# A recurrence, two expert layers and one core: the layout of its chunks in SBUF, its running products and its warming products

## The chip, the cores and the metric

The kernel runs on one core of a Trainium2 chip. The metric is the device time of one execution in microseconds. Three executions of the kernel before gave 916.23, 917.78 and 918.56 us, so the median is 917.78 us.

## The reference

For 4 batches of 8 heads a state of 48 by 48 is carried over 768 time steps with a complex gate for each row, and read by q:

```
mag = sqrt(a_re^2 + a_im^2);  scale = min(mag, 0.999) / (mag + 1e-6)
a_re, a_im = a_re * scale, a_im * scale                # B,H,S,D = 4,8,768,48
for t in range(S):
    S_re, S_im = ar*S_re - ai*S_im + k[t] v[t]^T, ar*S_im + ai*S_re
    y[t] = q[t] @ S_re
x = y as 3072 rows of 384
e = argmax(x @ w_gate + modality_bias[modality_id])     # one of 8 experts
x = gate_w * (relu(x @ w1[e]) @ w2[e])                  # 384 -> 1024 -> 384
out = (((x @ mid_w1) * (x @ mid_w2)) @ w3) @ w_out
```

## The kernel before, in words

**Stages.** First the gates are scaled. Then the recurrence is turned into products of matrices over chunks of CH = 128 time steps, 24 chunks of tokens with all their heads: the running product p(t) of the gates within a chunk is formed, q is multiplied by p(t) and k by 1/p(t). After that, for each chunk, TensorE forms scores (k times q, L1347), VectorE masks them with a causal triangle (L1253), and TensorE adds scores times v (L1397) and the state that came into the chunk (L1401). The rows then go through the gate and, sorted by expert, through the expert layers and the second layer, which is TensorE work from about 388 us to the end.

**The running products.** The gates of all batches lie in `gates[P, 2, NG, ROW]`: 128 partitions, real and imaginary plane, NG = 12 groups, and in a row 6 chunks of PITCH = 130 words. A chunk is worked on as two halves of SUB = 64 steps at once, so that a loop of 63 steps does for all (`for u in range(SUB - 1)`, L1052). In step u VectorE multiplies the gate of step u + 1, both planes, by the running product of step u: L1056 by its real and L1057 by its imaginary part, 288 elements each into `prods`, and L1059 and L1060 combine the products into the new real and imaginary part, 144 elements each (12 groups, 6 chunks, 2 halves). L1059 and L1060 wait for the products, the next step for L1060. All stands on VectorE, one instruction behind the other.

**The layout before.** The host interleaves the halves (`by_step`): word 2j + h of a chunk is step j of half h, so that the two words that a step touches in a chunk are neighbours. Two pad words end a chunk. Row p of a tile of tokens is therefore token `(p % 2) * 64 + p // 2` of its chunk (`when`), for the mask, for v, for the modality ids and for the token numbers that go with the sorted rows.

**The joins.** Two stages per batch (`stages`, 12 and 6 of its 18 chunk rows) finish a chunk: `join` (L1070 on) multiplies the second half by the last product of the first. Its steps 0 and 1 issue two instructions each at L1080 (real plane, imaginary plane), step 2 combines (L1084, L1085) and copies the last word to the pads (L1089 for the first stage, L1091 for the others). `norm` and `finish` then form 1/p from |p|^2, with Square, Ln and Exp on ScalarE (L878, L883, L888), and multiply in k (L1119, L1122, L1124) and q (L1136, L1127, L1129).

**What sets the order.** Everything is written out by hand. VectorE does the joins and finishes of the first two stages before the chunk loop, and the later ones between the chunks (`prepare(b, slot)`). SyncE's queue copies the finished planes into `ks` and `qs` (`stack_k`, `stack_q`, L753 and L724), which the scores read. TensorE, before the loop, forms w3 times w_out (L1326, L1331), then waits for the first half of k (`k_half_ready`, given by L1122) and runs 8 products of constants (`keep_busy`, L1318) until `ks` and `qs` are there.

Of the kernel before, what the change touches and what calls it, by code (L numbers as in the profile page):

```python
# [37 lines left out]
def constants(n_experts, n_tiles, n_steps, D, n_in, n_hidden):  # L38
# [10 lines left out]
    when = (row % 2) * SUB + row // 2  # L49
    put("causal", (when[:, None] <= when[None, :]) * 1.0)  # L50
# [14 lines left out]
    put("token", when[:, None] + CH * np.arange(n_tiles)[None, :])  # L65
# [535 lines left out]
def attention(nc, sem, io, shapes, L, R, W):  # L601
# [24 lines left out]
    with ExitStack() as room:  # L626
# [7 lines left out]
        def cst(name, rows=P):  # L634
# [4 lines left out]
            "p (w c n h) -> p w c n h", w=2, c=2, h=2)  # L639
# [68 lines left out]
        def plane(x, b):  # L708
            return gates[:, x, b * GB:(b + 1) * GB].rearrange("p g (c t) -> p (g c) t", t=PITCH)[:, :, 0:CH]
# [115 lines left out]
        def scalar(act):  # L825
            act.wait_ge(filled, 1)

            def re_square(b):
                act.wait_ge(gates_in[b][RE], landed(b))
                nc.scalar.activation(mags[b][:, :, :], plane(RE, b), ACT.Square).then_inc(re_squared, 1)  # L830

            def im_square(b):
                act.wait_ge(gates_in[b][IM], landed(b))
                nc.scalar.activation(squares[b], plane(IM, b), ACT.Square).then_inc(im_squared, 1)
# [39 lines left out]
            def square(k, x):  # L874
                b, part = stages[k]
                act.wait_ge(joined, k + 1)
                out = (norms[b], seeds[b])[x]
                nc.scalar.activation(out[:, part], plane(x, b)[:, part], ACT.Square).then_inc(p_squared, 1)  # L878
# [131 lines left out]
        def vector(dve):  # L1010
            def im_square(b):
                dve.wait_ge(gates_in[b][IM], landed(b))
                nc.vector.tensor_tensor(squares[b], plane(IM, b), plane(IM, b), ALU.mult).then_inc(im_squared, 1)
# [12 lines left out]
            def scale(b):  # L1026
# [4 lines left out]
                for x in (RE, IM):  # L1031
                    ins = nc.vector.scalar_tensor_tensor(out=plane(x, b), in0=mags[b][:, :, :], scalar=1.0, in1=plane(x, b),  # L1032
                                                         op0=ALU.subtract, op1=ALU.mult, reverse0=True)
# [30 lines left out]
            def join(k, step):  # L1064

                b, part = stages[k]
                half = gates[:, :, b * GB:(b + 1) * GB].rearrange("p x g (c j h) -> p x (g c) h j", j=SUB + 1, h=2)[:, :, part]
# [8 lines left out]
                if step < 2:  # L1076
                    last = half[:, step, :, 0, SUB - 1:SUB].broadcast_to([P, part.stop - part.start, SUB])
                    out = (by_re, by_im)[step]
                    for x in (RE, IM):
                        ins = nc.vector.tensor_tensor(out[:, x], half[:, x, :, 1, 0:SUB], last, ALU.mult)  # L1080
                    ins.then_inc(halves_done, 1)
                else:
# [4 lines left out]
                    if k == 0:  # L1087
                        pads = L.early_q[:, :, :, :].rearrange("p x g (c t) -> p x (g c) t", t=PITCH)[:, :, :, CH:PITCH]
# [15 lines left out]
            def finish(k, step):  # L1104
# [15 lines left out]
                elif step == 3:  # L1120
                    dve.wait_ge(kinv_ready, k + 1)
                    nc.vector.tensor_tensor(seed, inv, plane(RE, b)[:, part], ALU.mult).then_inc(k_half_ready, 1)  # L1122
                elif step == 4:
                    nc.vector.tensor_tensor(inv, inv, plane(IM, b)[:, part], ALU.mult).then_inc(kt_ready, 1)  # L1124
                elif step == 5:
                    dve.wait_ge(q_loaded, (b + 1) * DMA)
                    nc.vector.tensor_tensor(plane(RE, b)[:, part], plane(RE, b)[:, part], q_in[:, part], ALU.mult)  # L1127
                else:
                    nc.vector.tensor_tensor(plane(IM, b)[:, part], plane(IM, b)[:, part], q_in[:, part],  # L1129
                                            ALU.mult).then_inc(qt_ready, 1)  # L1130

            def early_q():
                dve.wait_ge(q_loaded, DMA)
                for x in (RE, IM):
                    out = L.early_q[:, x].rearrange("p g (c t) -> p (g c) t", t=PITCH)[:, :, 0:CH]
                    nc.vector.tensor_tensor(out, plane(x, 0)[:, parts[0]], q_in[:, parts[0]], ALU.mult).then_inc(q_early_ready, 1)  # L1136
# [164 lines left out]
        def tensor(pe):  # L1301
# [4 lines left out]

            def turn_y(g):
# [28 lines left out]
            keep_busy(8, bank_scores[0])  # L1336

            for g in range(CHUNKS + 1):
# [3 lines left out]
                if g < CHUNKS:  # L1342
# [45 lines left out]
                if g:  # L1388
# [3 lines left out]
                    for pair in range(HU // 2):  # L1392
# [6 lines left out]
                        if last:  # L1399
                            for i, out, wide in zip(heads, outs, (HALF, D)):  # L1400
                                mm = nc.tensor.matmul(out, state[:, i * D:i * D + wide],  # L1401
                                                      qs[before % NU][:, i, last * PITCH:last * PITCH + CH], start=False, stop=True)
# [21 lines left out]
def recurrence(nc, sem, io, shapes, L, R, W):  # L1424
# [10 lines left out]
    with ExitStack() as room:  # L1435
# [36 lines left out]
        def sync(sp):  # L1472
            with sp.If(general(sp)):
# [29 lines left out]
                for b in range(B):  # L1503
                    for h in range(2):
                        sp.dma_start(L.rows(b)[h:P:2, :, 0:DM], io["x_rows"][b * S:(b + 1) * S, :].rearrange(
# [632 lines left out]
```

## Time and profile before

| | |
|---|---|
| median of 3 runs | 917.78 us |
| the profiled execution | 917.5 us, span 915.7 us |
| TensorE matmuls, busy | 768.6 us (84%) |
| VectorE, busy | 496.7 us (54%), 963 instructions |
| ScalarE, busy | 331.2 us (36%) |
| granted TensorE clock, mean | 0.966 |

The span is the time from the first to the last recorded instruction. Busy shares are means over stages in which different engines set the pace. A line such as L1056 is a line of the kernel before; "rows" and "gates" in the names of the profile are the buffers `rows0` (where `prods` lies) and `gates`, "mags" holds `norms` and `seeds`, "spare" k and q as loaded. TensorE's passes of fp32 products are recorded one by one, so that 8 products show as 16 rows.

### The profile page before, as it was taken

To read this page: it belongs to the slowest core of one execution; us is meant where nothing else is said; L and a number is where in the kernel's file an instruction comes from. 1 tells how busy PE (TensorE), PEld (TensorE's weight loads), DVE (VectorE), ACT (ScalarE), POOL (GpSimd) and SP (SyncE) were. 2 spreads that over 40 slices of the span, in tenths; PEclk is the share of its full clock that TensorE was granted. 3 is DMA by queue.
4 is the path that set the end of the run, shared out by engine and by line. 5 is a ranking of instruction groups with operands and counts; after the bars stand their busy time and mean duration, and the time that the engine had idled before them with its cause. 6 is when DMAs were issued, how large, how long until landed. Compare 5 with 4: busy or idle time off the path is not lost.

```text
span 915.7 us, 11775 instructions
## 1 busy us (share of the span) xinstructions
PE 768.6 (84%) x4541; PEld 641.9 (70%) x4541; DVE 496.7 (54%) x963; ACT 331.2 (36%) x657; POOL 128.7 (14%) x127
## 2 busy tenths in 40 slices
PE   0029910399999999899999999999999999999995
PEld 0015500188888888787888888888989898988885
DVE  4999999999899975866453454341111111212010
ACT  6932100354545434534453452333122222223120
POOL 0201100000000032410000000013232222323231
PEclk9999965599999999999999999999999999999998
DMA  9982120456666656427423430160000000000000
GB/s 380 373 270 83 69 87 0 122 147 172 185 180 165 188 161 206 141 81 238 147 96 104 128 106 9 73 207 1 35 0 35 1 26 9 18 18 9 26 1 35
DMA packets 46756, 99.19 MB, mean 108 GB/s; under 512 B 11616, under 2 KB 29920, under 8 KB 44384
## 3 DMA queue, kind: packets, MB, share of 16 engines
q1 hardware_dynamic: 41056, 79.37, 28.3%
q0 software_dynamic: 5632, 18.94, 5.9%
q8 instruction: 40, 0.66, 0.3%
q14 instruction: 28, 0.23, 0.1%
HBM read 60.32 MB, written 18.94 MB: 87 GB/s over the span
## 4 chain that ended last, share of the span: by engine, by line
PE 69%; DVE 19%; DMA 3%; ACT 3%; issue 2%; SPq 2%; POOL 1%; DVEq 0%
PE moe_bank L557 17%; PE moe_bank L558 17%; PE moe_bank L559 17%; PE bank L1347 4%; DVE rows L1056 3%; DVE rows L1057 3%; PE bank L1381 3%; DVE gates L1059 2%; PE bank L1397 2%; PE bank L1313 2%; DVE gates L1032 2%; DVE gates L1060 2%; DMA gates<-a_im 1%; PE bank L1401 1%; PE bank L1353 1%
## 5 line engine op out<-in xcount | busy, mean ns | idle before, releaser
L1934 DVE TENSOR_TENSOR u_sb<-x_in,moe_bank 128x512 f32<-128x512 f32 x48 | 33.0, 688 | 229.1 <-PE moe_bank L559 229.1
L1772 POOL TENSOR_TENSOR hid_lo<-u_sb,hid_hi 128x512 fp32r<-128x512 f32 x48 | 62.4, 1299 | 357.9 <-ACT hid_hi L1829 357.9
L557 PE MATMUL moe_bank<-xT_hi,w_hi 128*128 128x512 f32 x264 | 104.8, 397 | 0.0
L558 PE MATMUL moe_bank<-xT_lo,w_hi 128*128 128x512 f32 x264 | 104.8, 397 | 0.0
L559 PE MATMUL moe_bank<-xT_hi,w_lo 128*128 128x512 f32 x264 | 104.0, 394 | 0.0
L1326 PE MATMUL bank<-early_w_out,early_w3T 128*128 128x384 f32 x128 | 45.4, 512 | 66.3 <-DMA early_w_out<-w_out 62.9
L1326 PEld LDWEIGHTS bank<-early_w_out,early_w3T 128*128 128x128 f32 x128 | 24.9, 199 | 86.3 <-issue 65.0
L1848 ACT COPY x_in<-moe_bank 128x512 f32<-128x512 f32 x48 | 28.1, 586 | 143.7 <-PE moe_bank L559 143.7
L559 PE MATMUL moe_bank<-w_hi,hid_lo 128*128 128x384 f32 x192 | 64.5, 336 | 0.0
L557 PE MATMUL moe_bank<-w_hi,hid_hi 128*128 128x384 f32 x192 | 64.4, 335 | 0.0
L558 PE MATMUL moe_bank<-w_lo,hid_hi 128*128 128x384 f32 x192 | 64.4, 335 | 0.0
L559 PEld LDWEIGHTS moe_bank<-xT_hi,w_lo 128*128 128x128 f32 x264 | 49.9, 189 | 11.8
L557 PEld LDWEIGHTS moe_bank<-xT_hi,w_hi 128*128 128x128 f32 x264 | 49.5, 187 | 12.1 <-DVE hid_lo L552 0.4
L558 PEld LDWEIGHTS moe_bank<-xT_lo,w_hi 128*128 128x128 f32 x264 | 49.7, 188 | 11.5
L1318 PE MATMUL bank<-consts 128*128 128x512 f32 x16 | 9.7, 772 | 56.3 <-DVE mags L1122 56.3
L559 PE MATMUL moe_bank<-xT_hi,m_lo 128*128 128x512 f32 x144 | 56.8, 394 | 0.0
L557 PE MATMUL moe_bank<-xT_hi,m_hi 128*128 128x512 f32 x144 | 56.7, 393 | 0.0
L558 PE MATMUL moe_bank<-xT_lo,m_hi 128*128 128x512 f32 x144 | 56.6, 393 | 0.0
L1347 PE MATMUL bank<-qs,ks 96*128 96x128 f32 x384 | 55.4, 287 | 1.3 <-DMA qs<-gates 1.3
L1347 PEld LDWEIGHTS bank<-qs,ks 96*128 96x128 f32 x384 | 46.6, 191 | 9.2 <-issue 7.7
L557 PE MATMUL moe_bank<-hid_hi,w_hi 128*128 128x512 f32 x128 | 51.0, 398 | 0.0
L558 PE MATMUL moe_bank<-hid_lo,w_hi 128*128 128x512 f32 x128 | 50.2, 393 | 0.0
(219 smaller groups left out, 1641.1 us busy)
## 6 DMA issues: line engine op xcount, KB each, us to landing
stage<-w SPq DMA_DIRECT2D x10, 1536.0 KB, 8.3
ks<-mags SPq DMA_DIRECT2D x48, 144.0 KB, 2.8
x_sorted<-early_zero POOLq DMA_DIRECT2D x8, 772.0 KB, 21.9
qs<-gates SPq DMA_DIRECT2D x40, 146.2 KB, 2.7
gates<-a_re SPq DMA_DIRECT2D x4, 1170.0 KB, 12.3
gates<-a_im SPq DMA_DIRECT2D x4, 1170.0 KB, 14.7
x_in<-x_sorted SPq DMA_DIRECT2D x24, 193.0 KB, 3.0
spare<-k SPq DMA_DIRECT2D x4, 1152.0 KB, 5.4
```

Of the source, the lines that this page charges most:

```text
L557: nc.tensor.matmul(out, l_hi, r_hi, start=first, stop=False)
L558: nc.tensor.matmul(out, l_hi, r_lo, start=False, stop=False)
L559: return nc.tensor.matmul(out, l_lo, r_hi, start=False, stop=last)
L1032: ins = nc.vector.scalar_tensor_tensor(out=plane(x, b), in0=mags[b][:, :, :], scalar=1.0, in1=plane(x, b), op0=ALU.subtract, op1=ALU.mult, ...
L1056: nc.vector.tensor_tensor(prods[:, 0], at[:, :, :, u + 1], re, ALU.mult)
L1057: nc.vector.tensor_tensor(prods[:, 1], at[:, :, :, u + 1], im, ALU.mult).then_inc(products, 1)
L1326: mm = nc.tensor.matmul(psum[f % 2][:, 0:DM], L.w3T[:, k, f * P:(f + 1) * P], L.w_out[:, k], start=(k == 0), stop=True, skip_group_check=True)
L1347: mm = nc.tensor.matmul(bank_scores[g % 2][:, i * CH:(i + 1) * CH], ks[m][:, i, c * CH:(c + 1) * CH], qs[m][:, i, c * PITCH:c * PITCH + CH ...
L1381: mm = nc.tensor.matmul(bank_s[0:SD, i * WIDE:(i + 1) * WIDE], krs[last % 2][:, i], v_flat[:, at:at + WIDE], start=(last == 0 and i == 0), ...
L1772: nc.gpsimd.tensor_tensor(hid_lo[:, f], u_sb[:, f % 2], hid_hi[:, f].bitcast(F32), ALU.subtract).then_inc(u_lo_ready, 1)
L1848: nc.scalar.copy(a_sb[:, f % 2], bank_a[f % 2][:, :]).then_inc(a_ready, 1)
L1934: nc.vector.tensor_tensor(u_sb[:, f % 2], a_sb[:, f % 2], bank_b[f % 2][:, :], ALU.mult).then_inc(u_ready, 1)
```

## The change

**Layout.** The host no longer interleaves. A chunk is its two halves in the order of time, each followed by one pad word (64 + 1 + 64 + 1 words, 130 as before), so row p of a tile is token p of its chunk. `plane` gives runs of 64 words where it gave runs of 128, and `halved` and `of_halves` bring the other operands into the same shape. The word that step u touches is now alone: 144 words per plane, 65 words (260 bytes) apart. The scores and the state products read `qs` as two runs of 64 (`chunk_of_q`).

**One instruction for the products.** The products by the real and by the imaginary part become one instruction of 576 elements with both operands broadcast. In a join the two planes of step 0 become one instruction, and so do those of step 1.

**Six warming products** in place of eight.

```
-    when = (row % 2) * SUB + row // 2
-    put("causal", (when[:, None] <= when[None, :]) * 1.0)
+    put("causal", (row[:, None] <= row[None, :]) * 1.0)
...
         def plane(x, b):
-            return gates[:, x, b * GB:(b + 1) * GB].rearrange("p g (c t) -> p (g c) t", t=PITCH)[:, :, 0:CH]
+            return gates[:, x, b * GB:(b + 1) * GB].rearrange("p g (r t) -> p (g r) t", t=SUB + 1)[:, :, 0:SUB]
+
+        def halved(a):
+            return a.rearrange("p c (h t) -> p (c h) t", h=2)
+
+        def of_halves(part):
+            return slice(2 * part.start, 2 * part.stop)
...
-            at = gates[:, :, :, :].rearrange("p x g (c j h) -> p x (g c) j h", j=SUB + 1, h=2)
+            at = gates[:, :, :, :].rearrange("p x g (r j) -> p x (g r) j", j=SUB + 1)
+            both = [P, 2, 2, NG * BLK]
             for u in range(SUB - 1):
-                re, im = (at[:, x:x + 1, :, u].broadcast_to([P, 2, NG * NCH, 2]) for x in (RE, IM))
                 if u:
                     dve.wait_ge(prefix_step, u)
-                nc.vector.tensor_tensor(prods[:, 0], at[:, :, :, u + 1], re, ALU.mult)
-                nc.vector.tensor_tensor(prods[:, 1], at[:, :, :, u + 1], im, ALU.mult).then_inc(products, 1)
+                nc.vector.tensor_tensor(prods, at[:, :, :, u + 1].unsqueeze(1).broadcast_to(both),
+                                        at[:, :, :, u].unsqueeze(2).broadcast_to(both), ALU.mult).then_inc(products, 1)
                 dve.wait_ge(products, u + 1)
                 nc.vector.tensor_tensor(at[:, RE, :, u + 1], prods[:, 0, 0], prods[:, 1, 1], ALU.subtract)
                 nc.vector.tensor_tensor(at[:, IM, :, u + 1], prods[:, 0, 1], prods[:, 1, 0],
                                         ALU.add).then_inc(prefix_step, 1)
...
-                half = gates[:, :, b * GB:(b + 1) * GB].rearrange("p x g (c j h) -> p x (g c) h j", j=SUB + 1, h=2)[:, :, part]
+                half = gates[:, :, b * GB:(b + 1) * GB].rearrange("p x g (c h j) -> p x (g c) h j", j=SUB + 1, h=2)[:, :, part]
...
-                    last = half[:, step, :, 0, SUB - 1:SUB].broadcast_to([P, part.stop - part.start, SUB])
+                    last = half[:, step:step + 1, :, 0, SUB - 1:SUB].broadcast_to([P, 2, part.stop - part.start, SUB])
                     out = (by_re, by_im)[step]
-                    for x in (RE, IM):
-                        ins = nc.vector.tensor_tensor(out[:, x], half[:, x, :, 1, 0:SUB], last, ALU.mult)
-                    ins.then_inc(halves_done, 1)
+                    nc.vector.tensor_tensor(out, half[:, :, :, 1, 0:SUB], last, ALU.mult).then_inc(halves_done, 1)
...
-                        pads = L.early_q[:, :, :, :].rearrange("p x g (c t) -> p x (g c) t", t=PITCH)[:, :, :, CH:PITCH]
+                        pads = L.early_q[:, :, :, :].rearrange("p x g (c h j) -> p x (g c) h j", j=SUB + 1, h=2)[:, :, :, :, SUB]
...
+            def chunk_of_q(m, i, c):
+                return qs[m][:, i, c * PITCH:(c + 1) * PITCH].rearrange("p (h t) -> p h t", h=2)[:, :, 0:SUB]
...
-            keep_busy(8, bank_scores[0])
+            keep_busy(6, bank_scores[0])
...
-                        mm = nc.tensor.matmul(bank_scores[g % 2][:, i * CH:(i + 1) * CH], ks[m][:, i, c * CH:(c + 1) * CH],
-                                              qs[m][:, i, c * PITCH:c * PITCH + CH], start=True, stop=True)
+                        mm = nc.tensor.matmul(bank_scores[g % 2][:, i * CH:(i + 1) * CH].rearrange("p (h t) -> p h t", h=2), ks[m][:, i, c * CH:(c + 1) * CH],
+                                              chunk_of_q(m, i, c), start=True, stop=True)
...
-        chunks = np.pad(by_step(a).reshape(P, -1, S // CH, CH), ((0, 0), (0, 0), (0, 0), (0, 2)))
-        return np.ascontiguousarray(chunks).reshape(P, -1, S // CH * (CH + 2))
+        halves = np.pad(packed(a).reshape(P, -1, S // SUB, SUB), ((0, 0), (0, 0), (0, 0), (0, 1)))
+        return np.ascontiguousarray(halves).reshape(P, -1, S // SUB * (SUB + 1))
```

On VectorE, the last step of the running products, the first two stages' joins and what stands between them, in the kernel before ("rows" is `prods`; the numbers are partitions and free sizes of what is written):

```order
L1056 TENSOR_TENSOR rows<-gates 128x288
L1057 TENSOR_TENSOR rows<-gates 128x288
L1059 TENSOR_TENSOR gates<-rows 128x72x2
L1060 TENSOR_TENSOR gates<-rows 128x72x2
L1080 TENSOR_TENSOR mags<-gates 128x12x64 x4
L1084 TENSOR_TENSOR gates<-mags 128x12x64
L1085 TENSOR_TENSOR gates<-mags 128x12x64
L1089 COPY early_q<-gates 128x24x2
L1136 TENSOR_TENSOR early_q<-gates,spare 128x12x128 x2
L1098 SCALAR_TENSOR_TENSOR mags<-mags 128x1536
L1102 TENSOR_REDUCE guard<-mags 128x1
L1080 TENSOR_TENSOR mags<-gates 128x6x64 x4
```

And the same piece after the change (its lines have moved: L1061 is the products, L1064 and L1065 combine them, L1084 is the join):

```order
L1061 TENSOR_TENSOR rows<-gates 128x576
L1064 TENSOR_TENSOR gates<-rows 128x144
L1065 TENSOR_TENSOR gates<-rows 128x144
L1084 TENSOR_TENSOR mags<-gates 128x2x12x64 x2
L1087 TENSOR_TENSOR gates<-mags 128x12x64
L1088 TENSOR_TENSOR gates<-mags 128x12x64
L1092 COPY early_q<-gates 128x48
L1140 TENSOR_TENSOR early_q<-gates,spare 128x24x64 x2
L1101 SCALAR_TENSOR_TENSOR mags<-mags 128x1536
L1105 TENSOR_REDUCE guard<-mags 128x1
L1084 TENSOR_TENSOR mags<-gates 128x2x6x64 x2
```

Nothing has changed its place; a step has three instructions where it had four, a join four where it had six, and the combining ones write 144 single words where they wrote 72 pairs.

On TensorE, the end of the work before the chunk loop and its first rows, before the change (L1318 is the warming product, L1347 the scores):

```order
L1331 MATMUL bank<-early_minus,consts 128x384 x2
L1318 MATMUL bank<-consts 128x512 x8
L1347 MATMUL bank<-qs,ks 128x128 x4
L1361 MATMUL bank<-qs,consts 96x24 x2
L1372 MATMUL bank<-consts,ks 128x96 x4
```

And after it (L1326 is the warming product, L1355 the scores):

```order
L1339 MATMUL bank<-early_minus,consts 128x384 x2
L1326 MATMUL bank<-consts 128x512 x6
L1355 MATMUL bank<-qs,ks 128x128 x4
L1369 MATMUL bank<-qs,consts 96x24 x2
L1380 MATMUL bank<-consts,ks 128x96 x4
```

Two warming products are gone; the rest stands as it was.

## Rows read from the trace of the kernel before

**Rows 1.** The page's part 4, shares of the chain by engine:
```profile
PE 69%; DVE 19%; DMA 3%; ACT 3%; issue 2%; SPq 2%; POOL 1%; DVEq 0%
```
**Rows 2.** Stretches: length; busy PE, PEld, DVE, ACT, POOL; clock, DMA share, GB/s:
```profile
64.08:153.84 89.76, 49.71 (x143) 27.01 (x141) 85.42 (x252) 11.17 (x24) 8.59 (x16) 0.82 0.21 75
153.84:184.54 30.70, 9.51 (x16) 4.10 (x17) 30.28 (x33) 9.09 (x8) 0.00 (x0) 0.57 0.41 100
184.54:352.87 168.33, 159.91 (x1630) 142.17 (x1628) 148.21 (x282) 83.15 (x223) 9.04 (x7) 1.00 0.62 169
```
**Rows 3.** VectorE in order of time, the first step; start us, duration us:
```profile
64.08 0.46 DVE L1056 TENSOR_TENSOR rows<-gates 128x288 f32<-128x288 f32 x1
64.45 0.45 DVE L1057 TENSOR_TENSOR rows<-gates 128x288 f32<-128x288 f32 x1
64.94 0.31 DVE L1059 TENSOR_TENSOR gates<-rows 128x144 f32<-128x144 f32 x1
65.17 0.30 DVE L1060 TENSOR_TENSOR gates<-rows 128x144 f32<-128x144 f32 x1
65.50 0.46 DVE L1056 TENSOR_TENSOR rows<-gates 128x288 f32<-128x288 f32 x1
```
**Rows 4.** VectorE by shape; busy us, mean ns of one, idle before:
```profile
L1056 DVE TENSOR_TENSOR rows<-gates 128x288 f32<-128x288 f32 x63 | 28.9, 458 | 2.2
L1059 DVE TENSOR_TENSOR gates<-rows 128x144 f32<-128x144 f32 x63 | 19.5, 309 | 2.2
L1080 DVE TENSOR_TENSOR mags<-gates 128x768 f32<-128x768 f32 x16 | 14.5, 948 | 0.0
```
**Rows 5.** VectorE by shape, reduces and one-source instructions, dense and strided:
```profile
L1022 DVE TENSOR_SCALAR mags<-mags 128x2304 f32<-128x2304 f32 x3 | 4.1, 1355 | 0.1
...
L254 DVE TENSOR_REDUCE route_c<-route_work 128x6 f32<-128x48 f32 x12 | 2.4, 200 | 0.3
...
L254 DVE TENSOR_REDUCE route_work<-part 128x48 f32<-128x192 f32 x3 | 1.4, 480 | 0.0
...
L1102 DVE TENSOR_REDUCE guard<-mags 128x1 f32<-128x12 f32 x4 | 0.7, 174 | 0.1
...
L254 DVE TENSOR_REDUCE route_c<-route_work 128x2 f32<-128x16 f32 x4 | 0.7, 167 | 0.1
L1102 DVE TENSOR_REDUCE guard<-mags 128x1 f32<-128x6 f32 x4 | 0.7, 163 | 0.1
...
L1091 DVE COPY gates<-gates 128x24 f32<-128x24 f32 x3 | 0.6, 191 | 0.1
...
L251 DVE TENSOR_SCALAR mod_f<-mod_f 128x24 f32<-128x24 f32 x2 | 0.4, 178 | 0.1
...
L254 DVE TENSOR_REDUCE route_work<-part 128x16 f32<-128x64 f32 x1 | 0.3, 267 | 0.0
...
L1089 DVE COPY early_q<-gates 128x48 f32<-128x48 f32 x1 | 0.2, 191 | 0.0
```
**Rows 6.** The chain in order of time, from 153 us: start us, us, what:
```profile
153.84 3.58 DVE mags L1080 x4
...
182.22 1.75 DVE mags L1080 x2
...
185.95 0.68 DVE scores L1253
```
**Rows 7.** TensorE's weight loads in order of time, in brackets the idle time before:
```profile
179.43 0.34 PEld L1318 LDWEIGHTS bank<-consts 128*128 128x128 f32 x1 [0.52 <-issue]
...
180.68 0.19 PEld L1318 LDWEIGHTS bank<-consts 128*128 128x128 f32 x1 [0.24 <-issue]
...
184.12 0.19 PEld L1347 LDWEIGHTS bank<-qs,ks 96*128 96x128 f32 x1 [0.24 <-issue]
```
**Rows 8.** SyncE's queue in order of time, the first planes of k:
```profile
174.91 6.23 SPq L753 DMA_DIRECT2D ks<-mags  x10
```
**Rows 9.** The transfers that write or read `ks`, 170 to 190 us:
```profile
DMA to landing us min/median/max: 2.2/2.8/3.2
```

More of the change, by code:

```diff
@@ L64, in constants @@
     put("region", one * (n_tiles * CH * np.arange(n_experts)))
-    put("token", when[:, None] + CH * np.arange(n_tiles)[None, :])
+    put("token", row[:, None] + CH * np.arange(n_tiles)[None, :])
     put("step", one * np.arange(n_steps))
@@ L829, in re_square @@
                 act.wait_ge(gates_in[b][RE], landed(b))
[L830 removed]
+                nc.scalar.activation(halved(mags[b][:, :, :]), plane(RE, b), ACT.Square).then_inc(re_squared, 1)
             def im_square(b):
                 act.wait_ge(gates_in[b][IM], landed(b))
[L834 removed]
+                nc.scalar.activation(halved(squares[b]), plane(IM, b), ACT.Square).then_inc(im_squared, 1)
             def root(b):
@@ L877, in square @@
                 out = (norms[b], seeds[b])[x]
-                nc.scalar.activation(out[:, part], plane(x, b)[:, part], ACT.Square).then_inc(p_squared, 1)
+                nc.scalar.activation(halved(out[:, part]), plane(x, b)[:, of_halves(part)], ACT.Square).then_inc(p_squared, 1)
             def log(k):
@@ L1012, in im_square @@
                 dve.wait_ge(gates_in[b][IM], landed(b))
-                nc.vector.tensor_tensor(squares[b], plane(IM, b), plane(IM, b), ALU.mult).then_inc(im_squared, 1)
+                nc.vector.tensor_tensor(halved(squares[b]), plane(IM, b), plane(IM, b), ALU.mult).then_inc(im_squared, 1)
             def add(b):
@@ L1031, in scale @@
                 for x in (RE, IM):
-                    ins = nc.vector.scalar_tensor_tensor(out=plane(x, b), in0=mags[b][:, :, :], scalar=1.0, in1=plane(x, b),
+                    ins = nc.vector.scalar_tensor_tensor(out=plane(x, b), in0=halved(mags[b][:, :, :]), scalar=1.0, in1=plane(x, b),
                                                          op0=ALU.subtract, op1=ALU.mult, reverse0=True)
@@ L1134, in early_q @@
                 for x in (RE, IM):
-                    out = L.early_q[:, x].rearrange("p g (c t) -> p (g c) t", t=PITCH)[:, :, 0:CH]
-                    nc.vector.tensor_tensor(out, plane(x, 0)[:, parts[0]], q_in[:, parts[0]], ALU.mult).then_inc(q_early_ready, 1)
+                    out = L.early_q[:, x].rearrange("p g (r t) -> p (g r) t", t=SUB + 1)[:, :, 0:SUB]
+                    nc.vector.tensor_tensor(out, plane(x, 0)[:, of_halves(parts[0])], halved(q_in[:, parts[0]]),
+                                            ALU.mult).then_inc(q_early_ready, 1)
             for step in range(3):
@@ L1400, in tensor @@
                             for i, out, wide in zip(heads, outs, (HALF, D)):
-                                mm = nc.tensor.matmul(out, state[:, i * D:i * D + wide],
-                                                      qs[before % NU][:, i, last * PITCH:last * PITCH + CH], start=False, stop=True)
+                                mm = nc.tensor.matmul(out.rearrange("p (h t) -> p h t", h=2), state[:, i * D:i * D + wide],
+                                                      chunk_of_q(before % NU, i, last), start=False, stop=True)
                     mm.then_inc(yT_psum, 1)
@@ L1504, in sync @@
                     for h in range(2):
-                        sp.dma_start(L.rows(b)[h:P:2, :, 0:DM], io["x_rows"][b * S:(b + 1) * S, :].rearrange(
+                        sp.dma_start(L.rows(b)[h * SUB:(h + 1) * SUB, :, 0:DM], io["x_rows"][b * S:(b + 1) * S, :].rearrange(
                             "(c h j) v -> h j c v", h=2, j=SUB)[h]).then_inc(rows_back, DMA)
@@ L2113 @@
     arrays = {
-        "a_re": spaced(a_re), "a_im": spaced(a_im), "k": by_step(k), "q_packed": by_step(q), "q": by_dim(q),
-        "v": np.ascontiguousarray(v.transpose(0, 2, 1, 3).reshape(NT, 2, SUB, H * D).transpose(2, 1, 0, 3)
-                                  ).reshape(CH, NT, H * D),
+        "a_re": spaced(a_re), "a_im": spaced(a_im), "k": packed(k), "q_packed": packed(q), "q": by_dim(q),
+        "v": np.ascontiguousarray(v.transpose(0, 2, 1, 3).reshape(NT, CH, H * D).transpose(1, 0, 2)),
         "a_re_d": by_dim(a_re), "a_im_d": by_dim(a_im), "k_d": by_dim(k),
```

17 lines of the change are left out of this document (8 added, 9 removed).

## The prediction

> **What bounds the kernel now.** I read the chain of waits first, since the change touches many lines and only those on the chain can move the end. TensorE holds 69% of it and VectorE 19% [rows 1]. The second view is the table of stretches: from 64.08 to 153.84 us VectorE is busy for 85.42 of 89.76 us, while TensorE does 49.71 us of other work that ends inside the stretch; ScalarE does 11.17 us and the DMA share is 0.21. After 184.54 TensorE is the full engine, 159.91 of 168.33 us [rows 2]. So the program has a VectorE part up to about 190 us and a TensorE part behind it, and every microsecond added to the VectorE part before the first scores moves everything behind it: the chunk loop cannot start without k and q, and nothing in it waits for anything else that is that early.
>
> The third view is the order of time on VectorE. In the running products the four instructions of one step start at 64.08, 64.45, 64.94 and 65.17, and the next step starts at 65.50 [rows 3]. The 63 steps end when the first join starts at 153.84 [rows 6]: (153.84 - 64.08) / 63 = 1.425 us per step. Nothing but VectorE itself stands between them.
>
> From these starts I take the cost of an instruction apart. 288 elements followed by an independent instruction take 0.37 to 0.38 us from start to start, 144 elements 0.23: about 1.04 ns an element and 0.075 us besides. Where the next instruction waits for the result, it is 0.49 for 288 and 0.33 for 144, so some 0.19 us besides. The means by shape agree: 458 ns for 288 elements and 309 for 144 give 1.035 ns an element, and a duration of 150 ns plus 1.04 ns an element gives 949 for 768, where 948 stands [rows 4].
>
> **The running products, if only the count of elements mattered.** Two instructions of 288 become one of 576 and the two of 144 stay. The new step is 576 x 1.04 + 190 = 0.789, then 0.225, then 0.335: 1.349 us, which is 0.076 less than 1.425, and 63 times that is -4.8 us. This is what the edit in the order of instructions is worth by itself.
>
> **The running products, with the new layout.** The other half of the edit is what the elements are. Before, the two halves of a chunk were interleaved, so each step read and wrote pairs of neighbouring words, one pair every 520 bytes. After, step u touches one word every 260 bytes. In these rows pairs pay nothing: 288 elements in pairs take 458 ns, where that formula gives 450 [rows 4]. Single words far apart are in the trace in three places [rows 5]:
> - The reduce of `part`, whose inner reads lie 32 bytes apart, takes 480 ns for 192 elements and 267 for 64: 1.66 ns an element. The reduces of the dense `route_work` take 200 ns for 48 and 167 for 16, 1.03 ns an element.
> - The reduce for `guard` reads one word every 512 bytes: 174 ns for 12 and 163 for 6, so 1.83 ns an element.
> - The one-source copy L1091 reads and writes one word every 520 bytes: 191 ns for 24 words, where a dense one-source instruction of 24 elements takes 178. Dense, such instructions run at (1355 - 178) / (2304 - 24) = 0.52 ns an element (L1022); the 13 ns more for 24 lone words add 0.54, so a lone word costs twice a dense one. At two elements side by side that is about 2.1 ns for each, which I round to 2.0. L1089 writes 48 words in pairs, each source word read twice, in 191 ns too: pairs pay nothing here either.
>
> So a lone word costs 1.66 to 2.0 ns where a dense one costs 1.04. What no row shows is a two-source instruction with both sources lone, nor a lone write with dense reads, which is what the two instructions that combine the products will do. I bound each:
> - The product instruction: 190 + 576 x 1.66, 1.83 or 2.0 = 1.146, 1.244 or 1.342 us from start to start, provided that the two source streams run beside each other as they do now. The lower bound is the 0.789 of the dense case; the upper one, if the two streams must take turns, is 190 + 576 x 3.66 = 2.298.
> - The two combining instructions: 0.56 us together if writes are free of it, 0.075 + 0.185 + 288 x r = 0.74, 0.79 or 0.84 if a lone write pays like a lone read. The copy L1091 has both kinds and cannot tell them apart.
>
> I take r = 1.83, since the reads of the `guard` reduce are the nearest in spacing and are read in the one-element-at-a-time form, and I take it for the writes too, because L1091, with lone reads and lone writes, pays the most of the three (2.0). The step is then 1.244 + 0.787 = 2.031 us, +0.606, and 63 steps are +38.2 us. Reads alone would be 1.244 + 0.56 = 1.804, +23.9 us.
>
> The Trainium skill speaks to this twice and the two passages pull apart. "Advanced Engine Details and Errata", section "SBUF Cachelines", says that SBUF works in lines of 16 bytes and that at least two hits on a line are needed to hide its latency; a pair is exactly two hits, a lone word one. The three places above agree with it. "VectorE: DVE Perf Modes", section "Mode 1× (REGULAR) — the baseline", says of the plain mode of two-source fp32 instructions that odd strides simply work in it, because nothing is packed; read as a promise of speed, it gives the -4.8 us of the dense case. The `guard` and `part` reduces read slower with stride here, so I give it little weight.
>
> **The joins.** Four instructions per join become two, each twice as long, so per join two gaps of 0.075 us go. Their halves are now dense runs of 64 where they were every second word; the row of every second word already runs at the dense price, 948 ns for 768 [rows 4], so the layout brings nothing there. On the chain before 190 us lie the four of the first join, the four of the second and two pairs of the third; the first four and the last pair stand in [rows 6]. That is six gaps, -0.45 us. The later joins lie beside TensorE's work; nothing.
>
> **The other layout edits.** Scaling and squares now work on 36 runs of 64 for 18 runs of 128, the matmuls that read `qs` on two runs of 64: the same elements, dense, 0. The pad copy of 48 words becomes lone writes, at most 48 x 0.5 = 24 ns, nothing. The constants, v and the modality ids are rearranged on the host at equal size.
>
> **Six warming products for eight.** Each has two passes, so sixteen in all. A weight load and the idle time before it make 0.34 + 0.52 = 0.86 us a pass at 179.43, and 0.19 + 0.24 = 0.43 at 180.68; the load for the first scores starts at 184.12 [rows 7]. In the stretch from 153.84 to 184.54 the mean granted clock is 0.57, and 1.00 after it [rows 2]: the passes run at 1.2 GHz first, and at 2.4 from somewhere between these two rows on. Six products are twelve passes, so four fast ones, 4 x 0.43 = 1.7 us, go: TensorE would be free at 184.5 - 1.7 = 182.8. The DMAs of `ks` are issued from 174.91 for 6.23 us [rows 8], and a landing takes 2.2 to 3.2 us more [rows 9], so the last lands between 183.3 and 184.3 and the scores could start there. It gains nothing, since VectorE is on the chain through the whole stretch and reaches its first mask at 185.95 [rows 6]. Bounds: -1 us (if the whole lead reached the end) to +1 us (if the clock fell in the short gap; passes of 0.86 in place of 0.43 for two microseconds). I take 0.
>
> **Sum.** The profiled execution took 917.5 us, of which the span is 915.7, against a median of 917.78. 917.5 + 38.2 - 0.45 = 955.3; on the median it would be 955.5. I say 955.4.
>
> **Rivals.**
> - Reads pay, writes do not. 917.8 - 0.45 + 17.7 (r = 1.66) to + 30.1 (r = 2.0): 935 to 947, at r = 1.83 941. For it: two of the three places show reads alone. Against: L1091 pays most. Chance 0.28.
> - No price for lone words in two-source instructions; the merged instruction saves its gap. 917.8 - 4.8 - 0.45 = 912.5, faster than before. It decides for the other side wherever a lone word costs less than 1.04 + 0.076 / 864 x 1000 = 1.13 ns, counted over all 864 elements of a step. For it: the rows of stride show reduces and copies only. Against: all three rows of it lie far above 1.13. Chance 0.10.
> - The two lone streams take turns: 2.298 + 0.787 = 3.085 us a step, +104.6, 1022 us. For it: in a step the two sources are neighbours, u and u+1. Against: today's pairs, two streams of them, pay nothing. Chance 0.05.
> - Between no price and the reads' price (913 to 935), a stream partly hidden: chance 0.07.
> - My forecast, reads and writes at 1.66 to 2.0 (+28.9 to +47.5): 946 to 965. Chance 0.50.
>
> The range for 8 in 10 leaves out the faster case and the case of turns, with edges for the sizes: 930 to 972. A difference under 0.3% (2.8 us) can't be told from none here. Faster 0.10, same 0.02, slower 0.88.
>
> **What would show it.** In the profile after, the 576-element instruction has a mean duration near 150 + 576 x 1.83 = 1204 ns (750 if only counts matter); the combining ones 410 ns for 144 elements if writes pay, 300 if not; the running products last 63 x 2.03 = 128 us where they last 90; the joins' rows show 1750 ns for 1536; the stretch from the first join to the last instruction stays as long as before within a microsecond. I am wrong if that stretch changes, or if the step stays under 1.43 us.

## The result, and the profile after

The changed kernel takes 949.35 us (median of 4 runs, 948.55 to 951.09) where the kernel before takes 917.0 us (4 runs of the same comparison): 1.0352 times as long, 95% interval 1.0334 to 1.0369. The forecast was 955.4 us in a range of 930 to 972. The profiled execution after took 949.5 us, its span is 947.7, 32.0 us more than before.

VectorE by shape in the kernel after (busy us, mean ns of one, idle before it):

```profile
L1061 DVE TENSOR_TENSOR rows<-gates 128x576 f32<-128x576 f32 x63 | 75.2, 1194 | 2.2
...
L1065 DVE TENSOR_TENSOR gates<-rows 128x144 f32<-128x144 f32 x63 | 26.5, 421 | 0.0
L1064 DVE TENSOR_TENSOR gates<-rows 128x144 f32<-128x144 f32 x63 | 26.4, 419 | 2.2
...
L1084 DVE TENSOR_TENSOR mags<-gates 128x1536 f32<-128x1536 f32 x8 | 13.9, 1750 | 0.0
...
L1092 DVE COPY early_q<-gates 128x48 f32<-128x48 f32 x1 | 0.2, 210 | 0.0
```

The one instruction of 576 lone words takes 1194 ns. The dense formula gives 150 + 576 x 1.04 = 749. The combining instructions have the same 144 elements as before and go from 309 to 419 ns [rows 4]: their sources are dense, only their writes have become lone. The pad copy of 48 words, once in pairs, goes from 191 [rows 5] to 210. The join of 1536 elements is dense and shows exactly the dense price.

VectorE in order of time, the first two steps after (start us, duration us):

```profile
64.21 1.20 DVE L1061 TENSOR_TENSOR rows<-gates 128x576 f32<-128x576 f32 x1
65.44 0.42 DVE L1064 TENSOR_TENSOR gates<-rows 128x144 f32<-128x144 f32 x1
65.69 0.42 DVE L1065 TENSOR_TENSOR gates<-rows 128x144 f32<-128x144 f32 x1
66.15 1.22 DVE L1061 TENSOR_TENSOR rows<-gates 128x576 f32<-128x576 f32 x1
```

And the stretches from the first step to the first join, from there to the first mask, and from there to the scatters ahead of the first expert block (length; busy PE, PEld, DVE, ACT, POOL; clock, DMA share, GB/s):

```profile
64.21:186.29 122.08, 47.43 (x139) 25.84 (x138) 117.75 (x189) 11.18 (x24) 8.59 (x16) 0.72 0.15 55
186.29:218.08 31.79, 10.53 (x37) 5.74 (x38) 31.34 (x30) 9.87 (x11) 0.00 (x0) 0.59 0.44 113
218.08:384.21 166.13, 157.66 (x1607) 139.77 (x1605) 146.05 (x270) 82.51 (x221) 9.05 (x7) 1.00 0.62 167
```

The running products last 122.08 us for 63 steps, 1.938 a step, where they lasted 89.76 [rows 2]. That is +32.3 us, the whole of the loss. From the first join to the first mask it was 185.95 - 153.84 = 32.11 us [rows 6] and is 31.79, and behind that nothing has changed that the profiles can tell: the last 729.6 us of the span (947.7 - 218.08) stand against 729.75 (915.7 - 185.95). That these two agree to 0.15 us is partly luck: in a second profile of the kernel before, the same stretch takes 733.3 us (919.2 - 185.94). The medians of the runs differ by 32.35 us.

The chain of waits after says the same: its VectorE share is 21% for 19% [rows 1], and the products' line leads all that is not in the expert layers.

```profile
PE 68%; DVE 21%; DMA 3%; ACT 3%; issue 2%; SPq 2%; POOL 1%; DVEq 0%
PE moe_bank L556 17%; PE moe_bank L557 17%; PE moe_bank L558 17%; DVE rows L1061 8%; PE bank L1355 4%; DVE gates L1064 3%; PE bank L1389 3%; PE bank L1405 2%; DVE gates L1065 2%; PE bank L1321 2%; DVE gates L1037 2%; DMA gates<-a_im 1%; PE bank L1409 1%; PE bank L556 1%; PE bank L557 1%
```

### The profile page after: what moved, and what is told of

The parts are those of the page before. It is cut to its first block, busy times and chain, and to the rows that moved or that the text cites. A ratio compares the mean times of both kernels' runs of the same rounds, so it can differ in the third digit from the quotient of the medians.

```text
span 947.7 us, 11688 instructions
## 1 busy us (share of the span) xinstructions
PE 769.1 (81%) x4537; PEld 642.6 (68%) x4537; DVE 527.7 (56%) x884; ACT 331.5 (35%) x657; POOL 128.1 (14%) x127
## 4 chain that ended last, share of the span: by engine, by line
PE 68%; DVE 21%; DMA 3%; ACT 3%; issue 2%; SPq 2%; POOL 1%; DVEq 0%
PE moe_bank L556 17%; PE moe_bank L557 17%; PE moe_bank L558 17%; DVE rows L1061 8%; PE bank L1355 4%; DVE gates L1064 3%; PE bank L1389 3%; PE bank L1405 2%; DVE gates L1065 2%; PE bank L1321 2%; DVE gates L1037 2%; DMA gates<-a_im 1%; PE bank L1409 1%; PE bank L556 1%; PE bank L557 1%
## 5 line engine op out<-in xcount | busy, mean ns | idle before, releaser
L1326 PE MATMUL bank<-consts 128*128 128x512 f32 x12 | 8.0, 832 | 90.7 <-DVE mags L1125 90.7
L1061 DVE TENSOR_TENSOR rows<-gates 128x576 f32<-128x576 f32 x63 | 75.2, 1194 | 2.2
L1326 PEld LDWEIGHTS bank<-consts 128*128 128x128 f32 x12 | 3.1, 272 | 95.3 <-issue 95.3
L1355 PE MATMUL bank<-qs,ks 96*128 96x128 f32 x384 | 55.5, 288 | 0.8 <-DMA qs<-gates 0.5
L1355 PEld LDWEIGHTS bank<-qs,ks 96*128 96x128 f32 x384 | 46.5, 191 | 9.1 <-issue 8.3
```

What stands on the lines that cost most here:

```text
L1061: nc.vector.tensor_tensor(prods, at[:, :, :, u + 1].unsqueeze(1).broadcast_to(both), at[:, :, :, u].unsqueeze(2).broadcast_to(both), ALU.m ...
```

## The experiments

**The products in two instructions again, layout as after.** It tells the spacing of the words from the form of the instruction.

```
-                nc.vector.tensor_tensor(prods, at[:, :, :, u + 1].unsqueeze(1).broadcast_to(both),
-                                        at[:, :, :, u].unsqueeze(2).broadcast_to(both), ALU.mult).then_inc(products, 1)
+                re, im = (at[:, x:x + 1, :, u].broadcast_to([P, 2, NG * BLK]) for x in (RE, IM))
+                nc.vector.tensor_tensor(prods[:, 0], at[:, :, :, u + 1], re, ALU.mult)
+                nc.vector.tensor_tensor(prods[:, 1], at[:, :, :, u + 1], im, ALU.mult).then_inc(products, 1)
```

> The kernel after, with the products of a step in two instructions of 288 again (by the real part, by the imaginary part); the layout of lone words and all else stay. Theory A, lone words (each of the 864 single words of a step costs more than a dense one, and merging saves one start): the two take 150 + 288 x 1.81 = 671 ns each, the step grows from 1.938 by 0.075 to 2.01 us, 63 steps are +4.7 us, so 954 us. Theory B, the form (the price lies in the instruction of 576 elements with both operands broadcast, not in the spacing): the two go back to 458 and 451 ns, the step to 1.938 - 1.23 + 0.865 = 1.57 us, -23 us, so 926 us.

Measured: 954.54 us (5 runs), 1.0411 times before, interval 1.0388 to 1.0434, so 5.2 us above the kernel after. VectorE by shape:

```profile
L1062 DVE TENSOR_TENSOR rows<-gates 128x288 f32<-128x288 f32 x63 | 42.4, 673 | 2.2
L1063 DVE TENSOR_TENSOR rows<-gates 128x288 f32<-128x288 f32 x63 | 42.0, 667 | 0.0
```

673 and 667 ns for instructions that differ from L1056 and L1057 of before only in the spacing of their words, 458 and 451 there: the spacing is the cost, not the form. The first join of its profile starts at 190.01 us and the first step at 63.97, so a step is 2.001 us, 0.063 above 1.938 where 0.075 was expected: merging is worth 63 x 0.063 = 4.0 us here. The other 1.2 us of the difference come later. In the profile VectorE idles 11.61 us in this kernel, and 5.09 in the kernel after, before the first copy of the expert steps (`x2T`). The run with merged joins below comes back to that place. The opposite case, one instruction for the products in the layout of pairs, was not run, so what the merge alone would give there is not shown.

**Instructions of one form, each by itself.** Between the scaling and the running products of the kernel before stand 14 groups of four VectorE instructions of 288 elements, with a wait behind each group. They write to a buffer that nothing reads afterwards. One group, with both sources lone:

```
+            for r in range(4):
+                nc.vector.tensor_tensor(out_dense(r), every(65, 1), every(65, 0), ALU.mult).then_inc(products, 1)
+            settle()          # waits for all four
```

> The kernel before with 14 groups of four VectorE instructions of 288 elements ahead of the running products, two fp32 sources, written to a buffer that nothing reads afterwards; a wait stands only behind each group. Dense: 450 ns and 0.375 us from start to start. Theory A (a lone word costs about 1.81 ns on either side): one source lone every 260 bytes 670 ns, both lone 670 (the streams run beside each other) and not 290 + 288 x 2.6 = 900; every 256 bytes the same as 260; reads every 32, 20 and 16 bytes 670, every 8 bytes 450, every 12 bytes between; pairs every 520 bytes 450; dense reads with lone writes every 32 or 16 bytes 560 to 670, every 8 bytes 450; both reads and writes lone 670, not their sum. Theory C (reads cost, writes are free): the lone writes 450. Theory D (256 bytes is worse than 260, that is banks and not lines): 256 over 700. The time of the run is that of the kernel before and some 30 us for the added instructions.

The one execution took 946.30 us. VectorE in order of time; L1072 is dense, the others in the order of the table below:

```profile
64.13 1.57 DVE L1072 TENSOR_TENSOR early_spare<-gates 128x288 f32<-128x288 f32 x4
65.73 2.39 DVE L1075 TENSOR_TENSOR early_spare<-gates 128x288 f32<-128x288 f32 x4
68.15 2.45 DVE L1078 TENSOR_TENSOR early_spare<-gates 128x288 f32<-128x288 f32 x4
70.64 2.98 DVE L1081 TENSOR_TENSOR early_spare<-gates 128x288 f32<-128x288 f32 x4
73.66 2.44 DVE L1084 TENSOR_TENSOR early_spare<-gates 128x288 f32<-128x288 f32 x4
76.13 2.46 DVE L1087 TENSOR_TENSOR early_spare<-gates 128x288 f32<-128x288 f32 x4
78.63 2.45 DVE L1090 TENSOR_TENSOR early_spare<-gates 128x288 f32<-128x288 f32 x4
81.11 1.93 DVE L1093 TENSOR_TENSOR early_spare<-gates 128x288 f32<-128x288 f32 x4
83.08 1.57 DVE L1096 TENSOR_TENSOR early_spare<-gates 128x288 f32<-128x288 f32 x4
84.68 1.57 DVE L1099 TENSOR_TENSOR early_spare<-gates 128x288 f32<-128x288 f32 x4
86.28 1.57 DVE L1102 TENSOR_TENSOR early_spare<-gates 128x288 f32<-128x288 f32 x4
87.88 2.26 DVE L1105 TENSOR_TENSOR early_spare<-gates 128x288 f32<-128x288 f32 x4
90.18 2.26 DVE L1108 TENSOR_TENSOR early_spare<-gates 128x288 f32<-128x288 f32 x4
92.47 2.46 DVE L1111 TENSOR_TENSOR early_spare<-gates 128x288 f32<-128x288 f32 x4
```

"Lone" is one word by itself, "every 260 B" the distance from one to the next. The last column is (time to the next group - 1.60) / 1152 elements, the mean over the group.

| line | sources | write | group to group, us | ns more per element |
|---|---|---|---|---|
| L1072 | dense | dense | 1.60 | - |
| L1075 | one lone every 260 B, one dense | dense | 2.42 | 0.71 |
| L1078 | both lone every 260 B | dense | 2.49 | 0.77 |
| L1081 | both lone every 256 B | dense | 3.02 | 1.23 |
| L1084, L1087, L1090 | both, every 32, 20, 16 B | dense | 2.47 to 2.50 | 0.76 to 0.78 |
| L1093 | both, every 12 B | dense | 1.97 | 0.32 |
| L1096 | both, every 8 B | dense | 1.60 | 0 |
| L1099 | both in pairs every 520 B | dense | 1.60 | 0 |
| L1102 | dense | every 8 B | 1.60 | 0 |
| L1105, L1108 | dense | every 16, 32 B | 2.30, 2.29 | 0.61, 0.60 |
| L1111 | both lone every 260 B | every 32 B | 2.49 | 0.77 |

Four things follow. Words 8 bytes apart, and pairs, are free; at 16, 20, 32 and 260 bytes the price is the same. Writes pay too, which refutes theory C. The two sources and the write do not add: the dearest stream sets the rate, 1.04 + 0.77 = 1.81 ns a word. And 256 bytes is dearer than 260, as theory D had it, but on top of the price of a lone word and not in its place.

The 0.60 for lone writes is less than the price of a word, since the dense group beside it has a start gap of 0.075 us between its instructions. Taken one by one, the instructions of L1105 start at 87.88, 88.39, 88.93 and 89.45, 0.52 us apart. The second and third of them, as one row:

```profile
88.39 1.23 DVE L1105 TENSOR_TENSOR early_spare<-gates 128x288 f32<-128x288 f32 x2
```

That is 1.81 ns for each of the 288 words and no gap besides.

**The second bench**, for the last of these: 12 groups in the same place, in the same form.

> As the first bench (groups of four VectorE instructions ahead of the running products; dense 1.60 us from one group to the next, both sources lone every 260 bytes 2.49, every 256 bytes 3.02). Theory A (the extra price at 256 bytes is one of banks: words a multiple of 256 bytes apart, or the two sources of one element, fall together): one source alone every 256 bytes also costs more than 2.42; every 512 bytes more than every 520 (144 elements each); every 64 and 192 bytes as 260. Theory B (it needs both sources): one source every 256 bytes 2.42, and with the sources 128 bytes apart 2.49 again. Lone writes of 144 elements every 32 and every 64 bytes cost the same, 0.075 + 144 x 1.64 = 0.31 us from start to start, or 0.25 as in the steps of the kernel after.

The one execution took 939.45 us.

```profile
64.06 1.57 DVE L1072 TENSOR_TENSOR early_spare<-gates 128x288 f32<-128x288 f32 x4
65.66 2.34 DVE L1075 TENSOR_TENSOR early_spare<-gates 128x288 f32<-128x288 f32 x4
68.03 3.00 DVE L1078 TENSOR_TENSOR early_spare<-gates 128x288 f32<-128x288 f32 x4
71.07 2.34 DVE L1081 TENSOR_TENSOR early_spare<-gates 128x288 f32<-128x288 f32 x4
73.45 2.45 DVE L1084 TENSOR_TENSOR early_spare<-gates 128x288 f32<-128x288 f32 x4
75.93 2.64 DVE L1087 TENSOR_TENSOR early_spare<-gates 128x288 f32<-128x288 f32 x4
78.60 2.42 DVE L1090 TENSOR_TENSOR early_spare<-gates 128x288 f32<-128x288 f32 x4
81.06 1.39 DVE L1093 TENSOR_TENSOR early_spare<-gates 128x144 f32<-128x144 f32 x4
82.48 1.67 DVE L1096 TENSOR_TENSOR early_spare<-gates 128x144 f32<-128x144 f32 x4
84.19 1.45 DVE L1099 TENSOR_TENSOR early_spare<-gates 128x144 f32<-128x144 f32 x4
85.67 1.20 DVE L1102 TENSOR_TENSOR early_spare<-gates 128x144 f32<-128x144 f32 x4
86.91 1.16 DVE L1105 TENSOR_TENSOR early_spare<-gates 128x144 f32<-128x144 f32 x4
```

One source every 256 bytes beside a dense one (L1075) takes 2.37 us a group, no more than at 260. Both every 256 bytes, one word apart, take 3.04 (L1078); the same with the second source 132 bytes away 2.38 (L1081). So the extra price at 256 bytes needs both sources: theory B. It is a matter of where the two lie to each other; by what mechanism is not shown. With both sources one word apart, every 192 and 64 bytes (L1084, L1090) take 2.48 and 2.46, like 260, but every 128 bytes (L1087) takes 2.67, which neither theory named. With 144 elements, every 512 bytes (L1096) takes 1.71 against 1.48 every 520 (L1099).

The last two groups are lone writes of 144, 32 and 64 bytes apart: 1.24 and 1.19 us. A quarter of that is 0.31 and 0.30, but it takes in the wait behind the group. Taken one by one, the instructions of L1102 start at 85.67, 85.93 and 86.19, 0.26 us apart, as in the steps of the kernel after (0.25). The last three and the middle two of them:

```profile
85.93 0.94 DVE L1102 TENSOR_TENSOR early_spare<-gates 128x144 f32<-128x144 f32 x3
86.19 0.69 DVE L1102 TENSOR_TENSOR early_spare<-gates 128x144 f32<-128x144 f32 x2
```

Between 144 and 288 lone writes lie 0.26 us from start to start, so 1.81 ns a word, and 1.82 by the groups (1.24 and 2.29 us). Between 144 and 288 elements with both sources lone (L1093 here, 1.42 us, and L1078 of the first bench, 2.49) it is 1.86. A lone write costs about what a lone read costs; only the start gap is missing.

**Eight warming products, all else as after.**

```
-            keep_busy(6, bank_scores[0])
+            keep_busy(8, bank_scores[0])
```

> The kernel after with eight warming products in place of six. Theory A: 0, within 0.5 us of the kernel after (949.3), since VectorE reaches its first mask after the scores are there in either case; the first scores start up to 1 us later. Theory B (TensorE's clock or its start matters): 1 us or more either way.

Measured: 948.54 us (5 runs), 1.0347 times before (1.0328 to 1.0366), against 1.0352 for the kernel after. The intervals lie on each other: the 0.8 us between the medians can't be told from nothing. TensorE's first scores and their weight loads with six products (kernel after):

```profile
215.51 0.68 PE L1355 MATMUL bank<-qs,ks 96*128 96x128 f32 x4 [0.33 <-DMA ks<-mags]
215.48 0.97 PEld L1355 LDWEIGHTS bank<-qs,ks 96*128 96x128 f32 x8 [1.13 <-issue]
```

And the first weight load for the scores with eight:

```profile
216.34 0.19 PEld L1355 LDWEIGHTS bank<-qs,ks 96*128 96x128 f32 x1 [0.24 <-issue]
```

With six, TensorE's weight loads pause for 1.13 us and its matmuls for only 0.33, until the transfer of `ks` has landed. The scores begin about 0.9 us sooner, and the granted clock is 1.00 in the gap and behind it (214.35 to 218.08 us). VectorE's first mask starts at 218.08 and 218.12 us in the two.

**The merged joins in the kernel before.**

```
-                    for x in (RE, IM):
-                        ins = nc.vector.tensor_tensor(out[:, x], half[:, x, :, 1, 0:SUB], last, ALU.mult)
-                    ins.then_inc(halves_done, 1)
+                    nc.vector.tensor_tensor(out, half[:, :, :, 1, 0:SUB], last, ALU.mult).then_inc(halves_done, 1)
```

> The kernel before with only the joins changed: steps 0 and 1 of a join in one instruction each, in the interleaved layout. Theory A: the merged ones take 1750 ns for 1536 elements, six gaps of 0.075 us go ahead of the first mask, -0.45 us, 916.6 for 917.0, and what lies beside TensorE brings nothing. Theory B (a merged instruction with three free dimensions and a broadcast runs slower): over 1750 ns and slower than before.

Measured: 918.53 us (11 runs) against 916.93, a ratio of 1.0015 (1.0003 to 1.0028): no gain where 0.45 us were expected, and the little that the intervals allow is a loss. The edit itself did as expected. First join and first mask in the chain:

```profile
153.77 3.44 DVE mags L1079 x2
...
185.56 0.68 DVE scores L1251
```

31.79 us between them, 32.11 before. The scatters ahead of the expert layers still start 1.3 us sooner, at 351.58 for 352.87. Then the chain has a transfer of weights that takes 6.65 us for 5.30 and so ends at the same time, and both kernels convert the first expert weights from 373.0 on. The loss comes behind that: at 418.24 us, where VectorE comes out of the recurrence block that it skips (a branch leads around it), this kernel waits for nothing that the profile shows, and longer:

```profile
418.24 1.29 DVE L1869 COPY x2T<-bank 128x512 f32 x2 [10.31 <-issue]
```

The kernel before, same copy:

```profile
412.98 1.29 DVE L1871 COPY x2T<-bank 128x512 f32 x2 [5.50 <-PE bank L559]
```

That is 5.3 us later for a copy on which the expert steps wait, and TensorE turns the rows of the next block at 450.25 us for 448.61, 1.6 us later. The chain of waits of the kernel with merged joins runs through this idle time, in two pieces:

```profile
408.76 3.49 issue
412.31 5.16 issue
```

The chain of the kernel before does not; there a product of TensorE ends VectorE's idle time. So the profiles put the loss here. No run took the idle time away, so it is not shown by an experiment.

**The same with an empty instruction behind each merged one** (`+ dve.nop()`), to give the stream its old length.

> The kernel before with the joins merged, as in the run before, and one empty instruction behind each merged one, so that VectorE's stream has as many instructions as before. In the run without them the first mask came 0.3 us sooner after the first join but VectorE stood idle for 10.31 us where it leaves the skipped recurrence block, for 5.50 in the kernel before. Theory A (the place of that jump in the instruction stream sets how long the fetch behind it takes): the idle time goes back to about 5.5 us and the time to 916.6. Theory B (it is chance, or the merged form costs elsewhere): 918.5 again, with 10 us idle, or with 5.5 us idle and the loss elsewhere.

Measured: 919.21 us (12 runs), ratio 1.0016 (1.0000 to 1.0032), idle 10.9 us. To bring back the number of instructions is not enough.

**The kernel before, and the one with merged joins, once more.**

> The kernel before once more, for the idle time of VectorE where it leaves the skipped recurrence block: 5.50 us in its first profile. Theory A (that time belongs to the program): 5 to 6 us again. Theory B (it changes from one execution to the next, and with it the time by 1 to 2 us): it may be 10 us here.

> The kernel before with merged joins once more: 10.31 us idle at that place in its first profile, 10.9 with empty instructions added. Theory A: about 10 us again, and the time 918 to 919. Theory B: it may be 5 us here, and the time then under 917.

Measured: 920.99 and 921.57 us, one run each on one chip, where the kernel before gave 920.91. The idle time before the copy is 5.3 us in the first and 9.7 in the second. In two profiles of each program it thus goes with the program and not with the execution, theory A; what in the program sets it stays open. In the kernel after it is 5.09 us, in the one with split products 11.6. The times are 0.6 us apart and both above what was expected. One run of each can't tell what the idle time costs.

**GpSimd takes the running products of the last batch, or of the last two.** Both from the kernel before.

```
+            late = gates[:, :, ND:NG].rearrange("p x g (c j h) -> p x (g c) j h", j=SUB + 1, h=2)
...
+                    nc.gpsimd.tensor_tensor(prods_pool[:, 0], late[:, :, :, u + 1], re, ALU.mult)
...
-            at = gates[:, :, :, :].rearrange("p x g (c j h) -> p x (g c) j h", j=SUB + 1, h=2)
+            at = gates[:, :, 0:ND].rearrange("p x g (c j h) -> p x (g c) j h", j=SUB + 1, h=2)
```

> The kernel before with the running products of the last batch (3 of 12 groups) on GpSimd, which is idle there; VectorE's products are 216 elements, its combining ones 108. If a step on VectorE costs 1.04 ns an element and 0.525 us besides, it goes from 1.425 to 0.525 + 648 x 1.04 = 1.20 us, -14.2 us, so 903 us. Rival: the two engines share a way to SBUF, and VectorE's instructions grow while GpSimd runs; with 63 steps of GpSimd at some 1.3 us this would take back part or all of the 14 us. Second rival: the steps of GpSimd stand between its stores of w3 x w_out, so that TensorE's early work ends late, after the first k: then the gain ends there.

> The same with the last two batches (6 of 12 groups) on GpSimd. If a step costs as above: 0.525 + 432 x 1.04 = 0.97 us, -28.4 us, so 888.6 us. GpSimd needs about 63 x 1.8 = 113 us, from 64 to about 190, and the join of the third batch needs it at about 200; if GpSimd is slower than that, the chunk loop waits for it and the gain is less than in the run with one batch.

Measured: 921.68 us for one batch where 903 was expected (8 runs, ratio 1.0045, 1.0029 to 1.0061), and 944.57 for two where 888.6 was (5 runs, 1.0297, 1.0275 to 1.0320). VectorE and GpSimd by shape, one batch:

```profile
L1015 POOL TENSOR_TENSOR rows<-gates 128x72 f32<-128x72 f32 x63 | 29.7, 471 | 0.0
...
L1082 DVE TENSOR_TENSOR rows<-gates 128x216 f32<-128x216 f32 x63 | 28.2, 448 | 0.0
...
L1085 DVE TENSOR_TENSOR gates<-rows 128x108 f32<-128x108 f32 x63 | 23.8, 378 | 0.0
```

216 elements take 448 ns where they should take 375, and 108 take 378 for 262. The first join starts at 155.00 us, no sooner than with all on VectorE; with two batches 144 elements take 492 ns where 300 are due, and it starts at 176.56. The first rival holds, and the run with one batch shows it by itself. From 71.7 to 74.5 us GpSimd has no step to do (it waits to store w3 x w_out); there a step of VectorE takes 1.20 us, as was expected. With GpSimd's steps beside it, it takes 1.47:

```profile
72.77 0.38 DVE L1082 TENSOR_TENSOR rows<-gates 128x216 f32<-128x216 f32 x1
79.85 0.43 DVE L1082 TENSOR_TENSOR rows<-gates 128x216 f32<-128x216 f32 x1
```

The second combining instruction of a step (L1085) takes 0.27 us alone and 0.41 with GpSimd beside it. GpSimd is held up in turn. Its 72 elements take 0.36 us beside the steps and 0.6 to 1.95 beside VectorE's longer instructions from 155 to 188 us. Its steps last until 199 us, and VectorE's joins of 768 elements take 1000 ns on average for 948. No version here beats the kernel before.

## Why the prediction was right

**Where the time goes.** That the running products alone would move the end, one to one: right. 32.3 us there, -0.3 between first join and first mask, 32.0 in the span.

**The price of lone reads.** r = 1.83 was taken from the `guard` reduce; the bench and the kernel after show 1.81. That it is so close is partly luck: 174 and 163 ns are printed to 1 ns, which leaves 1.7 to 2.0, and the other two places gave 1.66 and 2.0. The instruction of 576 was to take 1204 ns and takes 1194. The streams run beside each other, as the pairs had suggested: one lone source costs 0.71, two 0.77.

**The price of lone writes.** That they pay at all was the weakest step, taken from one copy that could not tell reads from writes. It holds, in groups of the bench that have nothing else lone, and r was right for it too: 1.81 ns a word. What was mis-sized is the fixed part of that term, the gap of 0.075 us to the next, independent instruction. The two combining instructions were to take 0.787 us together and take (65.69 - 65.44) + (66.15 - 65.69) = 0.71. The second of these is 0.46 for 0.449, as forecast; the first is 0.25 for 0.338, with no room for a gap beside 144 x 1.81 = 260 ns. 63 times the difference of 0.077 us is 4.9 us of the 6 us by which the forecast was too high. The products are 1.23 for 1.244, 0.9 us more. The duration of 419 ns, forecast as 410, does not show this: the next, independent instruction starts 0.25 us after the first one, 0.17 us before the first one ends.

**The merge.** 0.075 us a step was expected, 0.063 measured in the layout of lone words.

**The joins.** Six gaps, -0.45 us: 0.32 between first join and first mask in the kernel after and in the run with merged joins alone. In the time of that run it does not show (918.53 us for 916.93).

**Warming.** 0 expected, none found, for the reason given: VectorE holds the first mask. TensorE's scores came 0.9 us sooner; the 1.7 us of four passes were cut short by the landing of `ks`, as the prediction had it.

**The rivals.** Reads alone (941): refuted by the lone writes of the bench. No price (912.5): refuted by 673 for 458 ns. Taking turns (1022): refuted at the spacing of this kernel by 0.77 for both sources against 0.71 for one; at 256 bytes two sources do cost more than one, 1.23 against 0.67. A stream partly hidden (913 to 935): the time lies outside.

**The two passages.** The Trainium skill, "Advanced Engine Details and Errata", section "SBUF Cachelines", has lines of 16 bytes and wants at least two hits on a line. The benches agree: 8 bytes apart free, 16 full price, 12 bytes, where half of the words are alone on their line, about half (0.32 of 0.77). The extra for two sources at 128, 256 and 512 bytes does not follow from it. The Trainium skill, "VectorE: DVE Perf Modes", section "Mode 1× (REGULAR) — the baseline", says that odd strides work in the plain mode. That is true of what works here, not of its speed: 673 ns for 458.

## What to carry to other kernels

Before merging small strided instructions, look at the spacing of their words. Two neighbours per touch, 8 bytes, cost nothing. One alone costs 1.7 times a dense one on VectorE (1.81 for 1.04 ns), in reads and writes, while a merge saves only one start of 0.06 to 0.08 us. The price could be read before the change from strided copies and reduces in the trace, within 1.66 to 2.0 ns, by the slope between two sizes and not by one duration. And a duration is not what an instruction costs the next one: look at the starts. This chain of small dependent VectorE instructions was not helped by giving a part to GpSimd.

## What the runs showed of the hardware beyond that

- Two sources of one VectorE instruction, each read every 256 bytes and one word apart, cost 1.23 ns more per element than dense, and 0.93 more every 128 bytes; at 260 bytes, or every 256 with the second 132 bytes away or one source alone, 0.67 to 0.77.
- VectorE starts independent instructions with lone writes 0.26 us apart for 144 words and 0.52 for 288, dense ones 0.23 and 0.37.
- GpSimd beside VectorE on fp32 two-source work: 216 elements on VectorE take 0.43 us for 0.38, a step of four instructions 1.47 us for 1.20.
- VectorE's idle time where it leaves a skipped block: 4.9 to 5.5 us in seven programs, 9.7 to 11.6 in three. What sets it is open.
